# The start of the arena's large tiles moved by 32 bytes, from 32 past a multiple of 64 bytes to a multiple of 64

## The reference

```
# 1 attention: 4 batches, 8 heads, 768 positions, head size 64; 4 sink keys and a window of 128
scores = scale * q @ k.T ; keep sinks and 0 <= pos_q - pos_k < 128 ; softmax ; a @ v
# 2 mixture of experts: x is [3072, 512]; 8 experts, 512 -> 1024 -> 512, one expert for each token
e_idx = argmax(x @ w_gate + modality_bias[modality_id]) ; gate = softmax(logits)[e_idx]
out = gate * (relu(x @ w1[e_idx]) @ w2[e_idx])
# 3 feed-forward: 512 -> 2048 -> 512
h = x @ w_in ; g = h * sigmoid(1.702 * h) ; out = g @ w_out
```

## Time and profile before

| | us |
|---|---|
| median of 3 runs | 1128.5 (1128.02 to 1129.54) |
| the profiled execution | 1129.37 |
| its span, first to last instruction | 1127.5 |
| TensorE busy in it | 1112.4 (99%) |
| VectorE, ScalarE, GpSimd busy | 423.6, 378.1, 324.4 |
| DMA moved | 92.04 MB |

### The profile page before, as it was taken

How to read it: one execution, slowest core, us unless ns; L and a number is a source line. 1 busy time by engine, 2 the same in 40 slices (tenths; PEclk the granted TensorE clock), 3 DMA queues, 4 the chain that set the end, 5 groups by cost and what they waited for, 6 DMA issues and landing times.

```text
span 1127.5 us, 18740 instructions
## 1 busy us (share of the span) xinstructions
PE 1112.4 (99%) x5952; PEld 942.6 (84%) x5953; DVE 423.6 (38%) x1089; ACT 378.1 (34%) x781; POOL 324.4 (29%) x441
## 2 busy tenths in 40 slices
PE   9999999999999999999999999999999999999998
PEld 8999999987888888888878888888888888888887
DVE  4666666675222234122363223223323222322222
ACT  3666666633222233212352222222222222222222
POOL 8898988646642212122120001001001001000100
PEclk9999999999999999999999999999999999999999
DMA  9999988246111133211141001001101000000100
GB/s 208 228 262 240 242 223 219 66 131 249 47 47 47 37 112 130 75 47 37 46 171 46 20 0 56 19 0 47 28 0 47 19 9 37 0 0 1 38 1 37
DMA packets 57392, 92.04 MB, mean 82 GB/s; under 512 B 7936, under 2 KB 32768, under 8 KB 57344
## 3 DMA queue, kind: packets, MB, share of 16 engines
q1 hardware_dynamic: 51584, 72.56, 24.1%
q0 software_dynamic: 5760, 18.89, 4.8%
HBM read 72.02 MB, written 19.41 MB: 81 GB/s over the span
## 4 chain that ended last, share of the span: by engine, by line
PE 91%; DVE 4%; issue 2%; ACT 2%; DMA 1%; ACTq 0%; DVEq 0%; POOL 0%; SPq 0%; POOLq 0%
PE psum L981 8%; PE psum L972 8%; PE psum L974 8%; PE psum L983 8%; PE psum L973 8%; PE psum L982 8%; PE psum L789 5%; PE psum L938 4%; PE psum L940 4%; PE psum L913 4%; PE psum L915 4%; PE psum L914 4%; PE psum L939 4%; PE psum L764 2%; PE psum L925 2%
## 5 line engine op out<-in xcount | busy, mean ns | idle before, releaser
L1643 DVE TENSOR_TENSOR g<-psum,g 128x512 f32<-128x512 f32 x96 | 66.3, 691 | 306.5 <-ACT g L1176 306.4
L1176 ACT ACTIVATE g<-psum 128x512 f32<-128x512 f32 x96 | 57.3, 597 | 319.2 <-PE psum L974 316.5
L972 PE MATMUL psum<-x2T,win_hi 128*128 (+1 forms) x384 | 153.1, 399 | 2.3 <-DVE g L1643 2.3
L981 PE MATMUL psum<-w_hi,gT_hi 128*128 128x512 f32 x384 | 153.2, 399 | 0.0
L974 PE MATMUL psum<-x2T,win_lo 128*128 (+1 forms) x384 | 152.4, 397 | 0.0
L973 PE MATMUL psum<-x2T,win_hi 128*128 (+1 forms) x384 | 152.1, 396 | 0.0
L983 PE MATMUL psum<-w_hi,gT_lo 128*128 128x512 f32 x384 | 150.4, 392 | 0.0
L982 PE MATMUL psum<-w_lo,gT_hi 128*128 128x512 f32 x384 | 149.3, 389 | 0.0
L721 POOL DMA_INDIRECT out<-o_out,out_rows x20 | 19.5, 973 | 424.7 <-ACT o_out L1189 420.1
L789 PE MATMUL psum<-v_sb,pT 128*128 128x73 f32 x704 | 105.9, 269 | 2.4 <-DVE pT L1397 1.2
L1385 DVE CUSTOM_DVE_ANT_0 s_msk<-psum,mask_sb 128x260 f32<-128x260 f32 (+1 forms) x192 | 75.0, 403 | 71.8 <-PE psum L753 39.3
(11 more groups left out here) (229 smaller groups left out, 1986.5 us busy)
## 6 DMA issues: line engine op xcount, KB each, us to landing
qk_raw<-qkT SPq DMA_DIRECT2D x64, 384.0 KB, 8.0
stage<-w SPq DMA_DIRECT2D x12, 1024.0 KB, 5.1
x<-y_rows SPq DMA_DIRECT2D x24, 256.5 KB, 2.6
vT_sb<-vT SPq DMA_DIRECT2D x16, 384.0 KB, 8.5
v_sb<-vP SPq DMA_DIRECT2D x16, 384.0 KB
x_rows<-x_sb SPq DMA_DIRECT2D x16, 384.0 KB, 4.0
win_raw<-w_in SPq DMA_DIRECT2D x16, 256.0 KB, 8.8
stage<-w_out SPq DMA_DIRECT2D x4, 1024.0 KB, 6.7
```

The costliest lines, as they stand in the source:

```text
L972: pe.matmul(bank, wh, hi, start=(c == 0), stop=False)
L981: pe.matmul(psum[:, OB[t], :], gh, hi, start=(f == 0), stop=False)
L1643: dve.tensor_tensor(g32[:, f % 2, :], psum[:, FB[f % 2], :], g32[:, f % 2, :], ALU.mult)\
```

## The change

One line rounds the mark up to 16 words (64 bytes) before the large tiles are placed.

```
-        ZW = top[0]
+        ZW = top[0] = -(-top[0] // 16) * 16
         w_hi = place("w_hi", [P, QUARTERS, QW], F32R)
         w_lo = place("w_lo", [P, QUARTERS, QW], F32R)
```

## The result

| | before | after |
|---|---|---|
| median, us | 1128.5 | 1118.38 (1117.51 to 1119.85, 5 runs) |
| ratio | | 0.9908, 95% interval 0.9897 to 0.9919 |
| profiled execution, us | 1129.37 | 1119.85 |
| its span, us | 1127.5 | 1117.9 |

The kernel is 10 us faster. The forecast was no change; the sign and most of the size are rival A's.

What follows compares the result with a forecast made beforehand. The prediction took TensorE, through the distance between its matmul starts, to bound the kernel from 254 us on. All terms were 0: 1129.4 us profiled, 0.9 above the median, gave 1128.5 us; range 1120 to 1135.

Steps and rivals of the forecast that it cites:

- rival A: L972 to L974 in stage 3: slower because moving and stationary operands lie unlike within 64 bytes; -7.5 us, 1121.0 us; chance 0.18.
- What bounds the kernel: From 254 us on, time is the count of TensorE matmuls times the distance between their starts; other engines wait for TensorE.
- The instructions of ScalarE, VectorE and GpSimd: Copies, splits and exponentials on moved tiles: taken as 0; GpSimd's key splits in the attention within 0.5 us either side.
- The attention's terms: Transposes of `probs` and products with `pT`, 1056 matmuls: taken as 0, bound 2.6 us to both sides.
- the DMAs: Transfers, chiefly `win_raw`, which moves but lands before its first reader: 0, up to 0.5 us either side.
- rival C: Something small in the attention from moved tiles: 1124.9 to 1132.1 us; chance 0.06 faster, 0.08 slower.
- matmuls of stages 2 and 3 ... I take 0: 3552 matmuls of 512 columns on TensorE: taken as 0, bounds -7.5 to +13.9 us.
- three spacings: Distances between matmul starts: 227.7 ns in stage 2, 234.2 in L972's blocks, 229.2 in L981's; forecast to stand.
- the score matmul: Attention's fp32r matmul with varying moving start: 192 durations within 273 to 290 ns, read as no large address effect.
- Rival B: Stage 2 and L981 to L983: moving operand's own start sets the distance; +13.9 us, 1142.4 us; chance 0.12.
- Rival D: Whole kernel: memory has no 64-byte unit that any engine meets; 1128.5 us, part of the 0.56 for no change.

## Why the prediction was wrong

*What bounds the kernel* held. TensorE's matmul distances were what the change could reach, and what moved the end. The instructions of ScalarE, VectorE and GpSimd that were watched are blind to these 32 bytes, as said; the changed kernel's lines answer to the earlier trace rows:

```profile
L1123 ACT CAST xsT_hi<-psum x26: 582/582/592, 253.7 to 553.1; 128x512 fp32r<-128x512 f32 x26
L1582 DVE TENSOR_TENSOR xsT_lo<-psum,xsT_hi x26: 683/693/694, 254.4 to 553.7; 128x512 fp32r<-128x512 f32 x26
L584 POOL TENSOR_TENSOR k_lo<-qk_raw,k_hi x31: 1809/1824/1837, 14.5 to 206.3; 128x768 fp32r<-128x768 f32 x31
```

The attention's terms, the DMAs and rival C: nothing, since the attention kept its 128.20 us in 130. These steps were right, or their bounds wide enough.

*The step that failed is the term "matmuls of stages 2 and 3 ... I take 0".* The prediction set two readings against each other and gave the weight to the wrong one. On one side stood three spacings that sorted by the places of the operands. On the other stood the score matmul, whose durations showed no second group. The trace of before and the runs show why that row could not speak on the case. First, its durations could not show the effect. Their ends are modelled, and they are the same with 128 columns as with 260:

```profile
60.25 0.28 PE L753 MATMUL psum<-k_lo,q_st 128*128 128x128 f32 x1
...
61.17 0.28 PE L753 MATMUL psum<-k_lo,q_st 128*128 128x260 f32 x1
```

A measure that misses 132 columns misses 6.5 ns too. The other side was carried by distances between starts. Besides:

- The row has at most 260 columns. The pair with 256 shows a turned sign and 2.5 ns instead of 6.5, so short streams say nothing on long ones.
- By the true unit hardly any of its starts is like: `k_lo` lies 128 bytes past `q_st` within 256, a head adds 96 and a block 16, so of 24 combinations of buffer and block one is a multiple of 256. That is 8 of the 192 steps. By the distance between starts, which the trace has, L753 stands 0.12 us ahead of the transposes behind it in these eight, and 0.12 in the middle of the others with 260 columns: no difference at this width that the trace can tell.

The term was put at 0 and measured -10.7 us by the blocks, about 8 in L972 to L974 and 2.7 in L981 to L983, which lies outside its lower bound of -7.5 as well. It is the whole gain of 10 us.

*Rival A* was right in its mechanism (the two operands against each other) and in the place. Of its price, the 1152 matmuls of L972 to L974 were put at 6.5 ns and -7.5 us, and measured 2.80 - 2.72 us a block, about 8 us in 96. What it lacked is the after-effect: it took the 229.2 ns of L981 to L983 as theirs. The run with `x2T` alone moved shows that they fall to 226.7 without a change to their own operands, 2.7 us more. With it, A would have read 1118, and the range, whose lower end was laid just under A's price, would have reached the measured time. Its condition "alike within 64 bytes" was too weak, and that it led to the right place was luck: here the 32 bytes also make the difference a multiple of 256.

*Rival B*, the moving operand's own start: `w_hi` came to where `x2T` lies within 128, and stage 2 took 5.03 us instead of 5.01, not the 5.15 of B. It falls. One argument against it was misread: `k_lo` passes this place for one head in four only in the first, second, fourth and sixth block of a head, not in each. *Rival D*, that no engine meets such a unit, falls too.

The sentence on the Trainium skill, page "SBUF — State Buffer", section "Who interferes with whom", is what the prediction set against A beside the score matmul: two independent read ports, and TensorE never waits on anyone. No run here tests whether other engines leave TensorE alone. The runs do show that TensorE is not indifferent to the places of its own two operands against each other: 2.72 or 2.80 us for the same 12 matmuls. That the two reads get in each other's way, as A had it, fits this, but no run shows it.

## What to carry to other kernels

Where TensorE is full, compare the distance between starts for blocks of equal matmuls before anything else; if one sort of block is some ns slower with no wait, compare the places of its two operands within 256 bytes, and move one tile alone to test it. One tile by 32 bytes was worth the whole change here. Don't carry "put both at the same place" as a rule: it holds for these streams of 512 fp32r columns and cost time at 256, so measure at the width that the kernel uses.

A natural experiment in a trace (a line whose address steps by itself) is evidence only where it has both groups by the unit in question, the same stream length, and a measure that could show the effect. Check first that the measure sees something known, such as half the columns.

## What the hardware showed that was not expected

- 12 matmuls of 512 fp32r columns take 2.72 us with starts that differ by a multiple of 256 bytes and 2.79 to 2.80 with 16, 32, 64 or 128 bytes of difference, in `x2T` against `win_hi`; 2.79 with 32 bytes in `gT` against `w_hi`.
- At 256 columns it is the other way round: 24 take 2.87 us like and 2.81 us unlike.
- A block of unlike operands leaves the next block, whose operands are like, 0.01 to 0.04 us longer, but not when the difference is 16 bytes. A block of 256-column matmuls does so too (2.74 to 2.75 us instead of 2.72), like or unlike.
- Left open: why the places of the two operands count at all, whether it is the load beside the stream or the matmul's own weights, why the sign depends on the length of the stream, and why one unlike load in three costs almost as much as three.
